# Moving per-head and per-batch vector work inside the attention stage of an attention and two-MoE kernel

## The chip, the cores and the metric

One Trainium2 chip, one of its cores. The metric is the device time of the kernel in microseconds; a run is one execution. The kernel before was run three times; one execution was profiled.

## The reference

Attention over q, k, v of shape [4 batches, 8 heads, 1152, 64] with queries pooled by two, and then two mixture-of-experts layers over the 2304 resulting rows of 512:

```python
q_pool = q.reshape(B, H, S // 2, 2, D).mean(axis=3)
scores = scale * np.matmul(q_pool, k.transpose(0, 1, 3, 2))
scores = scores - np.max(scores, axis=-1, keepdims=True)
attn = np.exp(scores)
attn = attn / (np.sum(attn, axis=-1, keepdims=True) + 1e-09)
x = rows(np.matmul(attn, v))                 # 2304 x 512, heads side by side
# layer 1: rows with x @ w_skip > 0 get x + gate * relu(x @ w1[e]) @ w2[e], e = argmax(x @ w_gate)
# layer 2: every row gets gate * sigmoid(x @ w_output_gate)[e] * relu(x @ w1[e]) @ w2[e]
```

Each layer has 8 experts of 1024 hidden units.

## The kernel before

The kernel has an attention stage over 32 heads (to about 575 us) and then two MoE stages that run tiles of 128 rows sorted by expert. The change is in the attention stage alone.

**Bodies.** Every engine runs one program order, `body(h)` for h from -2 to 32. In body h different heads are in different states: keys and queries of head h+2 are transposed and split into a high and a low part, the row maximum of head h+1 is found, the exact scores and exponentials of head h are made, and head h-1 is multiplied with the values, summed, transposed back and divided.

**PE (TensorE).** In body h, for each of nine key tiles t: `scores(h, t, half)` (L566, L567), and beside them the fifteen `prior(h+1, b)` blocks (L553), a coarse product of 384 columns whose maximum DVE takes. Priors use two banks in turn, so prior b waits until DVE has reduced block b-2. At t=0, 2 and 4 stand the twelve matmuls of `weighted(h-1, group)` (L583), at t=4 also `sums(h-1)`, at t=5 and 6 the transposes and small products back (L605, L611, L620), and at t=7 `trans_ql(h+1)` (L539, its transposes recorded at L501), which waits for `neg_max`. `ranks_of_batch(b)` (L632 to L641) counts, for a finished batch, how many rows go to each expert; it shares a bank with `weighted`, so `weighted` waits for routing step 8 (L579).

**ACT (ScalarE).** `exps(h, t)` (L848) after each score tile, the split of keys and queries, and, at t=7, after exp 7, the two copies `ql_out` (L859) that the next head's scores wait for.

**POOL (GpSimd).** `accumulate(h)` (L440, L443) adds the nine exponential tiles of head h in eight additions of 128x576, each after its exp, so that the additions of head h run partly during body h+1. After it, in the bodies named in SCATTER_IN, two indirect DMAs (`scatter_rows`, L457) send finished rows of a batch to memory.

**DVE (VectorE).** `pool_q(h+2)` (L1009), fifteen `block_max(h+1, b)` (L1035), between them `k_low` (L1015 to L1021: parts 0 and 1 after block 1, part 2 after block 5) and `q_low` (L1028, after block 7), then `negate_max(h+1)` (L1040) and `divide(h-1)`: den (L1048), reciprocal (L1050), tmpL (L1054), xrow (L1059) and, last, the addition of tmpL to the routing logits L (L1063). Each increments `norm`; five increments a head.

**Routing steps.** When a batch's eight heads are done (body RANKS_IN[b] = 9, 17, 25 for batches 0 to 2), eighteen small DVE steps (`route_step`, L1065) choose experts, gates and target rows. Each waits for the step ahead of it (`rt_chain`). RT_GAPS says where they stand: (late, place): [steps] is, in body RANKS_IN[b]+late, after block `place` (5 or 9; NBLK is the end of the body). Batch 3 has all its steps behind the last body. The names by line are: step 0 L1076 to L1078, 1 L1080 and L1082, 2 L1084, 3 L1088, 4 L1090, 5 L1093, 6 L1095, 7 L1097 and L1098, 8 L1102, 9 L1105 and L1106, 10 L1108 and L1109, 11 L1113, 12 L1115, 13 L1118, 14 L1121, 15 L1123, 16 L1125 and L1126, 17 L1128.

Of the kernel before, what the change touches and what calls it, by code (L numbers as in the profile page):

```python
# [5 lines left out]
def attention_moe_moe(nc, q, k, v, w_skip, w_gate1, w1a, w2a, w_gate2, w_ogate, w1b, w2b, out):  # L6
# [13 lines left out]
    PN = 128  # L20


    B, H, S, D = q.shape
    NH = B * H
# [3 lines left out]
    QT = -(-SQ // PN)  # L28
    Q_LAST = SQ - (QT - 1) * PN
    KB_ = 384  # L30
    NB = S // KB_
    NBLK = QT * NB
# [4 lines left out]
    TB = 2 * OJ  # L37
# [27 lines left out]
    with ctx:  # L65
# [156 lines left out]
        MXB, SB, OB, TR = 0, 2, 6, 7  # L222
# [38 lines left out]
        def tiles_of(ap, odd):  # L261
# [4 lines left out]
        RANKS_IN = [(b + 1) * H + 1 for b in range(B - 1)]  # L266
        RT_STEPS = 18
        RT_CHAIN = RT_STEPS - 1
        RT_GAPS = {(0, 5): [0], (0, 9): [1], (1, 5): [2, 3], (1, 9): [4], (2, 5): [5], (2, 9): [6, 7], (2, NBLK): [8],
                   (3, 5): [9], (3, 9): [10], (4, 5): [11, 12], (4, 9): [13, 14], (5, 5): [15], (5, 9): [16, 17]}  # L270
        SCATTER_IN = {at + 5 + n: (b, range(2 * n, 2 * n + 2)) for b, at in enumerate(RANKS_IN) for n in range(TB // 2)}

        def has(g):
            return 0 <= g < NH
# [224 lines left out]
        def _(pe):  # L499
            def transpose(o, i, n=PN):  # L500
                return nc.tensor.transpose(o, i, ident[0:n, 0:n])  # L501
# [31 lines left out]
            def trans_ql(g, j):  # L533
                u = g % 2
                if j == 0:
                    pe.wait_ge(neg_max, g + 1)
                for t in range(3 * j, min(QT, 3 * j + 3)):
                    o = (t % 3) * PN
                    last = transpose(PS[0:D + 1, MXB + j, o:o + PN], QLN[u][:, t, 0:D + 1])  # L539
                last.then_inc(qlt_done, 1)  # L540

            def prior(g, b):
# [28 lines left out]
            def weighted(g, group):  # L571

                u = g % 2
                if group == 0:
                    pe.wait_ge(v_in[u], 16 * nth(g))
                    wait(pe, norm, HEAD_NORM * (g - 1) + 3)
                    for b, at in enumerate(RANKS_IN):
                        if g == at + 2:
                            pe.wait_ge(rt_chain, b * RT_CHAIN + 9)  # L579
                pe.wait_ge(exp_done, KT * g + 3 * group + 3)  # L580
                for t in range(3 * group, 3 * group + 3):
                    for half in range(2):
                        last = nc.tensor.matmul(PS[64 * half:64 * half + D, OB, 0:HQ], Vt[u][:, t, :],  # L583
                                                P[u][:, t, half * HQ:(half + 1) * HQ],
                                                start=(t == 0), stop=(t == KT - 1))
                if group == 2:
                    last.then_inc(pv_done, 1)
# [58 lines left out]
            def body(h):  # L646

                now, after, before = has(h), has(h + 1), has(h - 1)
                blocks = iter(range(NBLK))
                for t in range(KT):  # L650
                    if t == 3 and has(h + 2):
                        trans_qh(h + 2, 0)
                    if now:
                        scores(h, t, 0)
                    if after and t < 7:
                        prior(h + 1, next(blocks))
                    if after and t < 7 and h <= 0:
                        keep_busy(1)
                    if now:
                        scores(h, t, 1)  # L660
                    if after and t < 7:
                        prior(h + 1, next(blocks))
                    if after and t < 7 and h <= 0:
                        keep_busy(2 if h < 0 else 1)
                    if t == 0:
                        if has(h + 2):
                            trans_k(h + 2, 0)
                            if h == FIRST:
                                keep_busy(14)
                        if before:  # L670
                            weighted(h - 1, 0)
                    if t == 1 and has(h + 2):
                        trans_k(h + 2, 1)
                        if h == FIRST:
                            keep_busy(5)
                    if t == 2 and before:
                        weighted(h - 1, 1)
                    if t == 3 and has(h + 2):
                        if h == FIRST:
                            keep_busy(5)  # L680
                        trans_qh(h + 2, 1)
                        if h == FIRST:
                            keep_busy(4)
                    if t == 4:
                        if before:
                            weighted(h - 1, 2)
                            sums(h - 1)
                        if after:
                            prior(h + 1, next(blocks))
                    if t == 5 and before:  # L690
                        back_values(h - 1)
                    if t == 6 and h - 2 in RANKS_IN:
                        ranks_of_batch(RANKS_IN.index(h - 2))
                    if t == 6 and before:
                        back_sums(h - 1)
                        back_logits(h - 1)
                    if t == 7 and after:
                        trans_ql(h + 1, 0)
                        trans_ql(h + 1, 1)
# [109 lines left out]
        def _(act):  # L809
# [101 lines left out]

            for h in range(FIRST, LAST):
                body(h)
                if h - 2 in RANKS_IN:
                    route_exps(RANKS_IN.index(h - 2))
            route_exps(B - 1)

            def route_acts(i):
# [56 lines left out]
        def _(dve):  # L975
# [67 lines left out]
            def divide(g):  # L1043

                T = PS[0:OP, TR, 0:OJ * PN].rearrange("p (j a d) -> p j a d", j=OJ, a=2)
                dve.wait_ge(out_done, g + 1)
                both = PS[0:OP, TR, OJ * PN:OJ * (PN + 2)]
                vec.tensor_scalar(den[:, :], both, 1e-9, None, ALU.add).then_inc(norm, 1)  # L1048
                dve.wait_ge(norm, HEAD_NORM * g + 1)
                vec.reciprocal(rden[:, :], den[:, :]).then_inc(norm, 1)  # L1050
                dve.wait_ge(norm, HEAD_NORM * g + 2)
                b, c = g // H, (g % H) * D
                by = rden[:, :].rearrange("p (j a) -> p j a", a=2).unsqueeze(3)
                vec.tensor_tensor(tmpL[:, :, :, :], PS[0:OP, OB, LOG:LOG + OJ * 2 * NL]  # L1054
                                  .rearrange("p (j a n) -> p j a n", j=OJ, a=2),
                                  by.broadcast_to([OP, OJ, 2, NL]), ALU.mult).then_inc(norm, 1)
                if b >= 2 and g % H == 0:
                    dve.wait_ge(rt_scat[b % 2], 16 * TB * (b // 2))
                vec.tensor_tensor(xrow[b % 2][:, :, c:c + D].rearrange("p (a j) d -> p j a d", a=2), T,  # L1059
                                  by.broadcast_to([OP, OJ, 2, D]), ALU.mult).then_inc(norm, 1)  # L1060
                dve.wait_ge(norm, HEAD_NORM * g + 3)
                Lb = L[:, b * TB:(b + 1) * TB, :].rearrange("p (a j) n -> p j a n", a=2)
                vec.tensor_tensor(Lb, Lb, tmpL[:, :, :, :], ALU.add).then_inc(norm, 1)  # L1063
# [78 lines left out]
                        ins.then_inc(w_lo[m], 1)  # L1142

            def body(h):
                routing = [(late, b) for b, at in enumerate(RANKS_IN) for late in range(6) if h == at + late]

                def route_in(place):
                    for late, batch in routing:
                        for n in RT_GAPS.get((late, place), ()):
                            route_step(batch, n)  # L1150
                if has(h + 2):
                    pool_q(h + 2)
                for b in range(NBLK):
                    if has(h + 1):
                        block_max(h + 1, b)
                    if has(h + 2):
                        if b == 1:
                            k_low(h + 2, 0)
                            k_low(h + 2, 1)
                        if b == 5:  # L1160
                            k_low(h + 2, 2)
                        if b == 7:
                            q_low(h + 2)
                    route_in(b)
                if has(h + 1):
                    negate_max(h + 1)
                if has(h - 1):
                    divide(h - 1)
                route_in(NBLK)
# [4 lines left out]
                body(h)  # L1174


            for done, n in enumerate([*range(8), *range(11, 17), 8, 9, 10, 17]):
                route_step(B - 1, n, done)

# [153 lines left out]
```

## Time and profile before

| | |
|---|---|
| runs | 1157.24, 1161.58, 1158.62 us; median 1158.62 |
| profiled execution | 1157.24 us, its span 1155.5 us |
| PE, DVE, ACT, POOL busy | 96%, 64%, 46%, 39% of the span |
| granted TensorE clock, mean | 0.983 |
| chain that ended last | PE 84%, DVE 5%, ACT 4% |

The span runs from the first to the last instruction; the time of a run lies a little above it. Times inside the profile are microseconds from the span's start. A row of a timeline gives start, length (from the first start to the last end for several, "x2"), engine, line, operation, and in brackets how long the engine stood idle before it and what released it. Successive DVE operations overlap in their records by about 0.08 us.

### The profile page before, as it was taken

What the parts mean: (1) busy time and instruction counts of PE and PEld (TensorE: products, weight loads), DVE (VectorE), ACT (ScalarE), POOL (GpSimd) and SP (SyncE); (2) the same over time, 40 slices, a digit from 0 to 9 for tenths busy, and PEclk for the clock granted to TensorE, in tenths of its full rate; (3) what the DMA queues carried; (4) which work ended last, traced back from release to release, by engine and by line L of the source; (5) the groups of instructions that cost most, each with busy time, mean ns of one, the idle gap of its engine ahead of it and who ended that gap; (6) DMA issues with size and microseconds to landing.
All of it is one profiled execution on the core that took longest, in us unless ns stands there. A gap on an engine that the chain in (4) does not pass through costs nothing.

```text
span 1155.5 us, 22128 instructions
## 1 busy us (share of the span) xinstructions
PE 1105.6 (96%) x7821; PEld 931.7 (81%) x7821; DVE 740.0 (64%) x1706; ACT 534.6 (46%) x945; POOL 454.1 (39%) x339
## 2 busy tenths in 40 slices
PE   7999999999999999999879999999799999999996
PEld 5777777777777777777578899988689999999995
DVE  7766667787678766776336777676545556555641
ACT  3555655555555555554323444443143534453320
POOL 0768876767876678666710000000000010000100
PEclk9999999999999999999989999999889999999999
DMA  5262225223332234211458214275492472141100
GB/s 128 65 225 73 62 73 145 63 73 86 76 87 72 63 86 100 68 47 38 158 176 319 111 37 174 79 268 185 174 341 91 157 277 97 38 172 36 46 10 14
DMA packets 74398, 132.61 MB, mean 115 GB/s; under 512 B 11040, under 2 KB 29472, under 8 KB 74320
## 3 DMA queue, kind: packets, MB, share of 16 engines
q10 hardware_dynamic: 26240, 69.22, 16.6%
q1 hardware_dynamic: 43424, 50.58, 16.4%
q0 software_dynamic: 4656, 11.79, 2.9%
q8 instruction: 46, 0.75, 0.3%
q14 instruction: 32, 0.26, 0.1%
HBM read 106.12 MB, written 19.24 MB: 108 GB/s over the span
## 4 chain that ended last, share of the span: by engine, by line
PE 84%; DVE 5%; ACT 4%; issue 2%; DMA 2%; ACTq 1%; POOL 1%; SPq 0%; DVEq 0%; POOLq 0%
PE PS L732 20%; PE PS L583 13%; PE PS L553 9%; PE PS L566 7%; PE PS L501 7%; PE PS L749 6%; PE PS L567 6%; PE PS L745 6%; PE PS L746 6%; ACT arena_p L848 2%; ACT QLT L859 2%; DVE W2L L1139 2%; PE PS L620 1%; PE PS L596 1%; PE PS L764 1%
## 5 line engine op out<-in xcount | busy, mean ns | idle before, releaser
L443 POOL TENSOR_TENSOR arena_a<-arena_a,arena_p 128x576 f32<-128x576 f32 x224 | 334.0, 1491 | 94.0 <-ACT arena_p L848 75.1
L1035 DVE TENSOR_REDUCE mx<-PS 128x1 f32<-128x384 f32 (+1 forms) x480 | 246.7, 551 | 120.6 <-PE PS L553 117.2
L732 PE MATMUL PS<-moe,W 128*128 128x128 f32 x2432 | 281.4, 277 | 2.2 <-ACT moe L934 2.2
L732 PEld LDWEIGHTS PS<-moe,W 128*128 128x128 f32 x2432 | 278.5, 193 | 4.6 <-ACT moe L934 2.8
L848 ACT ACTIVATE arena_p<-PS 128x576 f32<-128x576 f32 x288 | 187.6, 653 | 151.1 <-PE PS L567 150.3
L566 PE MATMUL PS<-QHT,KA 128*128 128x288 f32 x576 | 191.2, 335 | 7.6 <-ACT QLT L859 7.6
L553 PE MATMUL PS<-KA,QHT 128*128 128x384 f32 (+1 forms) x480 | 173.3, 362 | 2.1 <-DVE mx L1035 2.0
L567 PE MATMUL PS<-QLT,KB 65*128 65x288 f32 x576 | 168.8, 297 | 0.0
L820 ACT CAST W2H<-W2R 128x1024 fp32r<-128x1024 f32 x148 | 144.3, 1048 | 51.4 <-PE PS L749 40.7
L1139 DVE TENSOR_TENSOR W2L<-W2R,W2H 128x1024 fp32r<-128x1024 f32 x144 | 166.5, 1218 | 1.5 <-ACT W2H L820 1.5
L583 PE MATMUL PS<-arena_p,arena_a 128*64 128x288 f32 x1152 | 160.5, 414 | 0.0
L491 POOL DMA_INDIRECT out<-moe,oidx x23 | 22.8, 990 | 293.7 <-DVE moe L1299 293.7
L566 PEld LDWEIGHTS PS<-QHT,KA 128*128 128x128 f32 x576 | 109.3, 190 | 32.2 <-ACT QLT L859 14.9
L954 ACT ACTIVATE hTh<-PS 128x512 fp32r<-128x512 f32 x76 | 45.3, 597 | 191.1 <-PE PS L732 191.1
L745 PE MATMUL PS<-W2H,hTh 128*128 128x512 f32 x304 | 123.6, 406 | 1.4 <-ACT hTh L954 1.4
L746 PE MATMUL PS<-W2L,hTh 128*128 128x512 f32 x304 | 119.0, 392 | 0.0
L583 PEld LDWEIGHTS PS<-arena_p,arena_a 128*64 128x64 f32 x1152 | 74.4, 136 | 55.2 <-issue 16.8
L567 PEld LDWEIGHTS PS<-QLT,KB 65*128 65x128 f32 x576 | 109.3, 190 | 0.0
L474 POOL DMA_INDIRECT xs<-moe,tpu x16 | 18.0, 1124 | 225.7 <-DVE tpu L1258 225.7
L553 PEld LDWEIGHTS PS<-KA,QHT 128*128 128x128 f32 (+1 forms) x480 | 86.2, 180 | 25.3 <-issue 13.1
L749 PE MATMUL PS<-W2H,hTl 128*128 128x512 f32 x304 | 82.8, 394 | 2.4 <-DVE hTl L1218 2.4
L501 PE MATMUL PS<-ident,arena_a 128*128 128x128 f32 (+2 forms) x480 | 81.2, 278 | 3.7 <-DVE KA L1021 2.1
(174 smaller groups left out, 1174.1 us busy)
## 6 DMA issues: line engine op xcount, KB each, us to landing
W<-in_moe_w ACTq DMA_DIRECT2D x16, 2048.0 KB, 14.5
W2R<-in_moe_w ACTq DMA_DIRECT2D x16, 2048.0 KB
moe<-xs SPq DMA_DIRECT2D x40, 258.0 KB, 2.7
arena_a<-in_k SPq DMA_DIRECT2D x32, 288.0 KB, 2.9
arena_a<-in_v SPq DMA_DIRECT2D x32, 288.0 KB, 2.8
KB<-KA SPq DMA_DIRECT2D x32, 288.0 KB
arena_a<-in_q SPq DMA_DIRECT2D x32, 256.0 KB, 3.2
xs<-padrow SPq DMA_DIRECT2D x8, 258.0 KB, 3.2
```

Of the source, the lines that this page charges most:

```text
L443: nc.gpsimd.tensor_tensor(Acc[u], Acc[u], P[u][:, t, :], ALU.add).then_inc(acc_step, 1)
L501: return nc.tensor.transpose(o, i, ident[0:n, 0:n])
L553: nc.tensor.matmul(PS[0:n, MXB + b % 2, 0:KB_], QHT[g % 3][:, t * PN:t * PN + n], KA[g % 3][:, c * KB_:(c + 1) * KB_], start=True, stop=Tr ...
L566: nc.tensor.matmul(o, KA[g % 3][:, t * PN:(t + 1) * PN], QHT[g % 3][:, cols], start=True, stop=False)
L567: last = nc.tensor.matmul(o, KB[u][:, t * PN:(t + 1) * PN], QLT[u][:, cols], start=False, stop=True)
L583: last = nc.tensor.matmul(PS[64 * half:64 * half + D, OB, 0:HQ], Vt[u][:, t, :], P[u][:, t, half * HQ:(half + 1) * HQ], start=(t == 0), st ...
L732: last = nc.tensor.matmul(PS[:, HB + f // 4, (f % 4) * PN:(f % 4 + 1) * PN], W1[s][:, d, f * PN:(f + 1) * PN], xT[:, d, :], start=(d == 0) ...
L745: nc.tensor.matmul(PS[:, YB, 0:DM], hTh[:, f, :], W2H[s][:, f, :], start=(f == 0), stop=False)
L746: nc.tensor.matmul(PS[:, YB, 0:DM], hTh[:, f, :], W2L[s][:, f, :], start=False, stop=False)
L848: nc.scalar.activation(P[u][:, t, :].rearrange("p (a c) -> p a c", a=2), PS[:, b:b + 2, 0:HQ], ACT.Exp, scale=SCALE).then_inc(exp_done, 1)
L1035: vec.reduce_max(mx3[0:n, t, c:c + 1], PS[0:n, MXB + b % 2, 0:KB_], AX.X).then_inc(pr_max, 1)
L1139: ins = vec.tensor_tensor(W2L[s][:, f, :], W2R[s][:, f, :], W2H[s][:, f, :].bitcast(f32), ALU.subtract)
```

## The change

There are four edits, all in the attention stage.

1. `trans_ql` transposes the last query tile with its 64 real rows instead of 128.
2. The addition of a head's logits to L leaves `divide`, and becomes `add_logits(g)`; it runs one body later, after block 5 of the maxima (after `k_low` part 2 and ahead of the routing steps there). The last head's runs behind the last body, ahead of batch 3's steps.
3. The routing steps of batches 0 to 2 stand in four bodies instead of six; PE's ranks, its wait in `weighted` and ACT's `route_exps` come one body earlier.
4. The scatter pairs of a batch come two bodies earlier.

```diff
-        RT_GAPS = {(0, 5): [0], (0, 9): [1], (1, 5): [2, 3], (1, 9): [4], (2, 5): [5], (2, 9): [6, 7], (2, NBLK): [8],
-                   (3, 5): [9], (3, 9): [10], (4, 5): [11, 12], (4, 9): [13, 14], (5, 5): [15], (5, 9): [16, 17]}
-        SCATTER_IN = {at + 5 + n: (b, range(2 * n, 2 * n + 2)) for b, at in enumerate(RANKS_IN) for n in range(TB // 2)}
+        RT_GAPS = {(0, 5): [0], (0, 9): [1, 2, 3], (1, 5): [4, 5], (1, 9): [6, 7], (1, NBLK): [8], (2, 5): [9],
+                   (2, 9): [10], (3, 5): [11, 12], (3, 9): [13, 14, 15, 16, 17]}
+        SCATTER_IN = {at + 3 + n: (b, range(2 * n, 2 * n + 2)) for b, at in enumerate(RANKS_IN) for n in range(TB // 2)}
...
                 for t in range(3 * j, min(QT, 3 * j + 3)):
+                    n = PN if t < QT - 1 else Q_LAST
                     o = (t % 3) * PN
-                    last = transpose(PS[0:D + 1, MXB + j, o:o + PN], QLN[u][:, t, 0:D + 1])
+                    last = transpose(PS[0:D + 1, MXB + j, o:o + n], QLN[u][0:n, t, 0:D + 1], n)
...
                     for b, at in enumerate(RANKS_IN):
-                        if g == at + 2:
+                        if g == at + 1:
                             pe.wait_ge(rt_chain, b * RT_CHAIN + 9)
...
-                    if t == 6 and h - 2 in RANKS_IN:
-                        ranks_of_batch(RANKS_IN.index(h - 2))
+                    if t == 6 and h - 1 in RANKS_IN:
+                        ranks_of_batch(RANKS_IN.index(h - 1))
...
-                if h - 2 in RANKS_IN:
-                    route_exps(RANKS_IN.index(h - 2))
+                if h - 1 in RANKS_IN:
+                    route_exps(RANKS_IN.index(h - 1))
...
                                   by.broadcast_to([OP, OJ, 2, D]), ALU.mult).then_inc(norm, 1)
+
+            def add_logits(g):
+
+                b = g // H
                 dve.wait_ge(norm, HEAD_NORM * g + 3)
                 Lb = L[:, b * TB:(b + 1) * TB, :].rearrange("p (a j) n -> p j a n", a=2)
                 vec.tensor_tensor(Lb, Lb, tmpL[:, :, :, :], ALU.add).then_inc(norm, 1)
...
-                routing = [(late, b) for b, at in enumerate(RANKS_IN) for late in range(6) if h == at + late]
+                routing = [(late, b) for b, at in enumerate(RANKS_IN) for late in range(4) if h == at + late]
...
+                    if b == 5 and has(h - 2):
+                        add_logits(h - 2)
                     route_in(b)
...
+            add_logits(NH - 1)
             for done, n in enumerate([*range(8), *range(11, 17), 8, 9, 10, 17]):
                 route_step(B - 1, n, done)
```

## Rows read from the trace of the kernel before

**Rows 1.** The page, part 4: the chain that ended last, by engine.

```profile
PE 84%; DVE 5%; ACT 4%; issue 2%; DMA 2%; ACTq 1%; POOL 1%; SPq 0%; DVEq 0%; POOLq 0%
```

**Rows 2.** The timeline of all engines around the end of one head.

```profile
311.86 0.71 PE L501 MATMUL PS<-ident,arena_a 128*65 128x128 f32 x5
312.06 0.65 ACT L848 ACTIVATE arena_p<-PS 128x576 f32<-128x576 f32 x1 [1.11 <-PE PS L567]
...
312.57 0.30 DVE L1063 TENSOR_TENSOR L<-L,tmpL 96x150 f32<-96x150 f32 x1
312.61 0.68 ACT L859 CAST QLT<-PS 65x384 fp32r<-65x384 f32 x2
...
313.34 0.40 PE L566 MATMUL PS<-QHT,KA 128*128 128x288 f32 x1 [0.23 <-ACT QLT L859]
...
314.10 1.02 DVE L1035 TENSOR_REDUCE mx<-PS 128x1 f32<-128x384 f32 x2 [0.82 <-PE PS L553]
```

**Rows 3.** DVE's timeline over that head, with steps 0 and 1.

```profile
311.08 0.17 DVE L1040 TENSOR_REDUCE arena_a<-mx 128x5 fp32r<-128x15 f32 x1
...
319.37 0.28 DVE L1021 TENSOR_TENSOR KA<-PS,KA 64x128 fp32r<-64x128 f32 x1
319.69 0.20 DVE L1076 TENSOR_SCALAR do<-L 96x6 f32<-96x6 f32 x1
...
321.32 1.02 DVE L1035 TENSOR_REDUCE mx<-PS 128x1 f32<-128x384 f32 x2 [1.20 <-PE PS L553]
322.25 0.48 DVE L1028 TENSOR_TENSOR arena_a<-arena_a 128x320 fp32r<-128x320 f32 x1
...
323.59 0.53 DVE L1080 TENSOR_TENSOR gex<-L,gmx 96x96 f32<-96x96 f32 x1
...
325.34 1.59 DVE L1035 TENSOR_REDUCE mx<-PS 128x1 f32<-128x384 f32 x3 [1.05 <-PE PS L553]
...
328.20 0.17 DVE L1040 TENSOR_REDUCE arena_a<-mx 128x5 fp32r<-128x15 f32 x1
```

**Rows 4.** POOL's timeline, from four heads.

```profile
227.17 3.03 POOL L443 TENSOR_TENSOR arena_a<-arena_a,arena_p 128x576 f32<-128x576 f32 x2 [0.53 <-ACT arena_p L848]
...
234.16 1.44 POOL L443 TENSOR_TENSOR arena_a<-arena_a,arena_p 128x576 f32<-128x576 f32 x1
...
251.28 1.42 POOL L443 TENSOR_TENSOR arena_a<-arena_a,arena_p 128x576 f32<-128x576 f32 x1
...
318.43 1.42 POOL L440 TENSOR_TENSOR arena_a<-arena_p 128x576 f32<-128x576 f32 x1
...
322.31 1.69 POOL L443 TENSOR_TENSOR arena_a<-arena_a,arena_p 128x576 f32<-128x576 f32 x1 [0.90 <-ACT arena_p L848]
...
324.14 1.42 POOL L443 TENSOR_TENSOR arena_a<-arena_a,arena_p 128x576 f32<-128x576 f32 x1
```

**Rows 5.** DVE's timeline: routing steps in other heads and in the tail.

```profile
225.10 0.17 DVE L1040 TENSOR_REDUCE arena_a<-mx 128x5 fp32r<-128x15 f32 x1
...
227.33 1.60 DVE L1009 TENSOR_TENSOR arena_a<-arena_a 128x320 f32<-128x320 f32 x1
...
234.25 1.38 DVE L1106 TENSOR_TENSOR Racc<-Racc,Rsum 96x16 f32<-96x16 f32 x1
...
242.58 0.17 DVE L1040 TENSOR_REDUCE arena_a<-mx 128x5 fp32r<-128x15 f32 x1
...
251.48 1.24 DVE L1115 TENSOR_SCALAR gden<-gden 96x12 f32<-96x12 f32 x1
...
336.81 0.25 DVE L1084 TENSOR_TENSOR gc<-gc,rev 96x96 f32<-96x96 f32 x1
...
577.51 0.17 DVE L1115 TENSOR_SCALAR gden<-gden 96x12 f32<-96x12 f32 x1
```

**Rows 6.** PE's weight loads ahead of prior blocks 8 and 12.

```profile
321.93 0.19 PEld L553 LDWEIGHTS PS<-KA,QHT 128*128 128x128 f32 x1
...
325.95 0.13 PEld L553 LDWEIGHTS PS<-KA,QHT 128*64 128x64 f32 x1 [0.18 <-DVE mx L1035]
```

## The prediction

> **What bounds the kernel now.** The page comes first [rows 1]: on one core, the chain of work that ended last runs on PE for 84% of the span. The edits touch only the attention stage, up to about 575 us, so the next view is DVE's timeline. From one negate_max (L1040) to the next are 17.12 us [rows 3]. That period repeats through the stage, except for three heads of 17.48 us, which follow the ranks on PE (225.10 to 242.58, one of three) [rows 5]. So a routing step costs the kernel nothing today; only the rank matmuls cost 0.36 us a batch, and they stay.
>
> Next, what sets 17.12 us. At the end of a head [rows 2] PE issues scores(7) and then, from 311.86, the five transposes of trans_ql. ACT starts exp(7) at 312.06, released by scores(7), and starts the two QLT copies at 312.61, behind exp(7). The next head's first score waits for them until 313.34. This path runs through ACT, and the transposes are beside it. Inside a head PE issues without a break, with one stop: prior block 12 waits 0.18 us for the block maximum of block 10, the one that starts at 325.34 [rows 6]. Block 8 goes out at 321.93, when the maximum of block 6 (321.32, about 0.55 us long) has just ended at 321.87. At those two blocks DVE has no slack: what it is late there, PE is late, and nothing after it in the body gives time back. DVE's own room is ahead of them: 1.20 us idle before block maximum 6 with step 0 in it, 1.05 us before block maximum 10 with step 1 in it [rows 3]. These are the places (5) and (9) of the routing table.
>
> Last, POOL. Its adds of 1.42 us stand at fixed places in a head, as ACT's exps release them [rows 4]. Rows show what they do to DVE. Step 12 (L1115), 96x12, takes 1.24 us at 251.48, until POOL's add of 251.28 ends at 252.70; the same step took 0.17 us in the tail (577.51), where POOL is idle. L1009, 128x320 with two inputs, takes 1.60 us at 227.33, behind the add of 227.17; L1028, of the same size, takes 0.48. L1080 takes 0.53 us and ends when the add of 322.31 has ended; L1084, of the same size, takes 0.25 with no add beside it. The maxima, whose input lies in PSUM, never stretch [rows 3 to 5]. So a DVE operation with two SBUF inputs, or a copy or tensor_scalar in SBUF, stands still till the running add ends. Which side wins a tie is seen too: L1028 at 322.25 wins against the add of 322.31, which is stretched to 1.69 us; L1106 at 234.25 loses against the add of 234.16 and takes 1.38 us [rows 3 to 5].
>
> **The shorter transposes.** One of a head's five transposes has 64 columns instead of 128. The five take 0.47 us until the next LDWEIGHTS, 0.09 each; so the saving is 0 to 0.05 us a head [rows 2]. It lies ahead of scores(8), after which PE waits for QLT anyway: 0. Only in the first two heads does PE wait for L1040, so below 0.1 us in all.
>
> **The L addition moved from divide to place 5.** It leaves some 0.22 us of the head's end free (0.30 us less the overlap of 0.08). What follows on DVE is L1009 and then 0.82 us of idle time until PE's first prior [rows 2]: gain 0. In the tail it stands in the same place of the chain. At place 5 it starts when DVE is free of k_low(2), 319.37+0.28, so 8.61 us after L1040 with a gap of 0.04 us, like L1076 now. POOL's second add starts at 8.70 (251.28 - 242.58): L gets in ahead of it, ends at 8.9, and the room holds it in the 20-odd heads without routing. Cost 0; if it loses, it ends 0.18 us after the add's 10.12, which is 0.06 late.
>
> **The routing table.** Body at+n is body h = RANKS_IN[b] + n. I lay the steps on one head, times from L1040, with the slots that rows give [rows 3, 4]. Place 5 opens at 8.61, and block maximum 6 is due at 10.24. Place 9 opens at 12.51 and block maximum 10 is due at 14.26. POOL runs 8.8-10.2 (pushed a little by L), 11.23-12.9, 13.06-14.48, then nothing until 15.7. Gaps behind a wait are 0.04 us and an operation starts 0.08 us before the end of the one ahead if nothing separates them.
>
> Body at+0. Place 5: L, then step 0, whose first instruction waits for L and so comes at 8.95, into the second add. Released at 10.2, step 0 ends at 10.45, block maximum 6 starts at 10.39: 0.15 late. Then L1028 starts at 11.32, after POOL's third add (11.23): by the L1106 tie it loses, waits until about 12.65 and, with 0.34 after the release (L1009: 228.93 against 227.17 + 1.42), ends at 13.0. Block maxima 8 and 9 follow, 0.46 us each, still in time for priors 10 and 11, which have 1.7 us of room; place 9 opens at 13.85 instead of 12.51. POOL's fourth add, now 12.8-14.27, holds step 1. Steps 1, 2 and 3 then run freely, each about 0.25 (L1084) and 0.04: block maximum 10 starts at 15.03 instead of 14.26, **0.77 us late**. If L1028 wins instead, step 2 (L1084, two SBUF inputs) comes at 13.23, just after the fourth add, and is held to 14.48: then 0.55 at place 9 beside 0.1 at place 5, almost the same.
>
> Body at+1. L, then step 4 is held to 10.2 and step 5 waits for it: block maximum 6 is 0.29 late; L1028 loses; place 9 opens at 13.85 and takes step 6 (held to 14.27) and step 7 (two reduces): maximum 10 at 14.76, **0.50 late** over both places. Before, steps 6 and 7 fitted. Step 8 at the end is L1102 with L1009 behind it, as before.
>
> Body at+2. Step 9 behind L: L1105 held, maximum 6 0.09 late; step 10 alone at place 9: **0.10**.
>
> Body at+3. Steps 11 and 12: L1113 is a reduce, L1115 is held as now, no delay. Place 9 takes 13 to 17. Step 13 ends at 12.94, step 14 at 13.20, step 15 (L1123) comes at 13.24 and is held by the fourth add to 14.50; steps 16 and 17, at 0.17 an instruction by the tail's L1115, take 0.4 more: maximum 10 at 14.89, **0.63 late**, and 0.90 if L1028 loses here too (its margin is 0.06 us). I take 0.65.
>
> Sum: 0.77 + 0.50 + 0.10 + 0.65 = 2.02 us a batch, three batches, 6.06 us, less under 0.1 us of prologue: 6.0 us. Ends: 0 if these steps are never held (steps 2 and 3 would add 0.57 us to a room that has 1.05), and, if L1028 loses its tie in all four bodies and pushes the fourth add to end at 14.4, with the four bodies' steps behind that, 0.91 + 0.59 + 0.28 + 1.02 = 2.8 us a batch, 8.4 in all.
>
> One term hangs on whether step 0's L1076, a strided tensor_scalar, is held at all. The row leaves it open: 0.20 us at 319.69, POOL's add of that head ending at 319.85 [rows 3, 4]. I take it as held, like L1115, the nearest row; if it is not, body at+0 costs 0.55 and the sum is 5.3.
>
> The Trainium skill, "SBUF — State Buffer", section "SBUF: two separate sides", says that VectorE and GpSimd share a pair of SBUF ports under an exclusive lock, which an operation in a two-port mode or with two SBUF inputs takes for its whole length. By that rule L1076 is held too and the sum is the 6.0; by the other reading of the row it is 5.3. The trace agrees with the rule in L1115 and L1106.
>
> **Ranks, exps, scatters.** They keep their distance to the steps. PE's ranks still come after step 5 with 6 us to spare, route_exps still between steps 7 and 11. Scatter pairs move two bodies up. The pair in body 30, which stands in front of the last head's eight adds, is still there, only from another n: the last chain through POOL is not shortened. The pairs of bodies 31 and 32 vanish from beside the final divide, whose operations run at their usual lengths there today (L1063 0.30): under 0.1 us.
>
> **Rivals.**
> Hidden: DVE is not held, or PE makes it up. For: 1.05 and 1.20 us of idle time at the places, and no step now moves the 17.12. Against: the held rows and PE's 0.18 us wait at block 12. Time: 1157.2, chance 0.25.
> Slower: L1028 loses its tie in body at+3 too, and every step with a two-input operation meets an add. One mechanism, POOL's add ahead of DVE at q_low; it decides from 0.06 us of delay at block maximum 6. 8.4 us: 1165.6, chance 0.25. Against: L1115 alone ended in time for 252.82.
> Faster: the L addition and the transpose are on the path after all. 32 x (0.22 + 0.05) = 8.6 us: 1148.6. Against: both lie beside waits that end later; chance 0.03.
>
> **How the numbers follow.** The profiled execution took 1157.24 us (span 1155.5), the lowest of the three; their median is 1.4 above it. 1157.24 + 6.0 = 1163.2, chance 0.47, its own range 1161 to 1165. With the hidden and the held case the range is 1157 to 1166.5. A measurement tells about 0.5%, 5.8 us, from no change: from the median that is 1152.8 to 1164.4. Slower: the held case and a quarter of my own, 0.37. Faster 0.03. Same 0.60.
>
> **What would show it.** L1040 to L1040: 17.12 in bodies without routing; longer by about 0.8, 0.5, 0.1 and 0.65 in the four bodies of a batch (plus the ranks' 0.36 after at+1). L1084, L1123, L1090 and L1105 stretched beside a POOL add; L1028 at 1.5 us or more in at+0 and at+1; PE's idle time before block 12 rising from 0.18 to over 0.6; L1063 at 0.30. The prediction is wrong if PE's wait before block 12 stays at 0.18, or if L1063 itself is stretched in every head.

## The result and the profile after

The changed kernel takes 1163.89 us (median of 7 runs, 1162.94 to 1165.81) against 1158.59 us for the kernel before (7 runs, 1156.15 to 1161.58). The ratio is 1.0051, with a 95% interval of 1.0036 to 1.0065: slower, by 5.3 us between the medians and by 5.9 us by the ratio. The forecast was 1163.2 us with a range of 1157 to 1166.5. The profiled execution took 1163.63 us, its span 1161.9.

Where the time went is read from the starts of the 32 `negate_max` operations (L1040, now L1041), as for [rows 3]. From head 2 to head 31 they lie 496.87 us apart before (53.91 to 550.78) and 502.36 us apart after (53.93 to 556.29): 5.49 us in the attention stage. The rest of the span's 6.4 us lies behind it. The load of the first MoE stage's second tile of rows (L397, issued by SyncE) is issued at 599.11 before and 604.71 after, 5.60 us, and the remaining 0.8 us is within what single runs of either kernel differ by. All but 0.04 of the 5.49 us lies in the twelve bodies that hold routing steps; in the other heads from 3 to 30 the period is 17.11 to 17.14 us in both kernels.

First the page's part 4, the chain that ended last, to be set beside [rows 1]:

```profile
PE 82%; DVE 11%; issue 2%; DMA 2%; POOL 1%; SPq 0%; DVEq 0%; ACTq 0%; ACT 0%; POOLq 0%
```

ACT has left the chain (4% before) and DVE has 11% instead of 5%. Part of that is the real delay and part is a quirk of the head's end, told below.

DVE's timeline in the body at+0 of batch 0, to be set beside [rows 3] (lines have moved: negate_max is L1041, the maxima L1036, q_low L1029, L is added at L1068, step 0 is L1081 to L1083, step 1 L1085 and L1087, step 2 L1089, step 3 L1093):

```profile
173.82 0.17 DVE L1041 TENSOR_REDUCE arena_a<-mx 128x5 fp32r<-128x15 f32 x1
...
182.42 0.31 DVE L1068 TENSOR_TENSOR L<-L,tmpL 96x150 f32<-96x150 f32 x1
182.77 1.27 DVE L1081 TENSOR_SCALAR do<-L 96x6 f32<-96x6 f32 x1
...
184.19 1.00 DVE L1036 TENSOR_REDUCE mx<-PS 128x1 f32<-128x384 f32 x2
185.12 0.47 DVE L1029 TENSOR_TENSOR arena_a<-arena_a 128x320 fp32r<-128x320 f32 x1
...
187.18 1.35 DVE L1089 TENSOR_TENSOR gc<-gc,rev 96x96 f32<-96x96 f32 x1
188.57 0.25 DVE L1093 TENSOR_REDUCE gcm<-gc 96x12 f32<-96x96 f32 x1
188.74 1.57 DVE L1036 TENSOR_REDUCE mx<-PS 128x1 f32<-128x384 f32 x3
...
191.59 0.17 DVE L1041 TENSOR_REDUCE arena_a<-mx 128x5 fp32r<-128x15 f32 x1
```

POOL's adds beside it, as in [rows 4]:

```profile
182.52 1.49 POOL L443 TENSOR_TENSOR arena_a<-arena_a,arena_p 128x576 f32<-128x576 f32 x1
...
185.05 3.38 POOL L443 TENSOR_TENSOR arena_a<-arena_a,arena_p 128x576 f32<-128x576 f32 x2 [1.04 <-ACT arena_p L849]
```

The reader is to see three things. L1081, a 96x6 tensor_scalar, lasts 1.27 us and ends at 184.04, when the add of 182.52 has ended at 184.01. Step 2's L1089, a 96x96 product of 0.25 us, lasts 1.35. And where the row of block maximum 10 had 1.05 us of idle time in front of it before, here it has none: it starts 14.92 us after negate_max instead of 14.26. PE's weight loads ahead of prior block 12, in the bodies at+0, at+1 and at+3, tell what this costs, beside 0.18 in [rows 6]; the second row is prior block 8 in the body at+1:

```profile
189.34 0.13 PEld L554 LDWEIGHTS PS<-KA,QHT 128*64 128x64 f32 x1 [0.72 <-DVE mx L1036]
...
202.70 0.19 PEld L554 LDWEIGHTS PS<-KA,QHT 128*128 128x128 f32 x1 [0.23 <-DVE mx L1036]
...
206.91 0.13 PEld L554 LDWEIGHTS PS<-KA,QHT 128*64 128x64 f32 x1 [0.36 <-DVE mx L1036]
...
242.21 0.13 PEld L554 LDWEIGHTS PS<-KA,QHT 128*64 128x64 f32 x1 [0.81 <-DVE mx L1036]
```

In the body at+1 the delay comes in two parts: prior 8 goes out 11.11 us after negate_max instead of 10.84, 0.27 us late, and the wait at block 12 adds 0.18. The chain of holds is the longest there. DVE's timeline: step 4 (L1095) behind L, q_low (L1029) behind POOL's third add, and the two maxima behind q_low:

```profile
200.42 1.47 DVE L1095 TENSOR_TENSOR gc<-gc,gcm 96x96 f32<-96x96 f32 x1
...
203.03 1.55 DVE L1029 TENSOR_TENSOR arena_a<-arena_a 128x320 fp32r<-128x320 f32 x1
204.50 1.01 DVE L1036 TENSOR_REDUCE mx<-PS 128x1 f32<-128x384 f32 x2
```

The periods from one negate_max to the next, for the four bodies of batch 0 (batches 1 and 2 give the same to 0.03 us):

| body | before | after | after - before | forecast |
|---|---|---|---|---|
| at+0 | 17.12 | 17.77 | +0.65 | +0.77 |
| at+1 | 17.12 | 17.57 | +0.45 | +0.50 |
| at+2 | 17.11 | 17.54 | +0.07 and the ranks' 0.36, which came one body later before | +0.10 |
| at+3 | 17.48 | 17.76 | +0.64 without that 0.36 | +0.65 |

These sum to 1.81 us a batch, 5.4 in three.

### The profile page after: what moved, and what is told of

Its sections match the earlier page's. It is cut to its first block, busy times and chain, and to the rows that moved or that the text cites. A ratio compares the mean times of both kernels' runs of the same rounds, so it can differ in the third digit from the quotient of the medians.

```text
span 1161.9 us, 22128 instructions
## 1 busy us (share of the span) xinstructions
PE 1116.4 (96%) x7821; PEld 934.7 (80%) x7821; DVE 752.0 (65%) x1706; ACT 537.6 (46%) x945; POOL 451.3 (39%) x339
## 4 chain that ended last, share of the span: by engine, by line
PE 82%; DVE 11%; issue 2%; DMA 2%; POOL 1%; SPq 0%; DVEq 0%; ACTq 0%; ACT 0%; POOLq 0%
PE PS L733 20%; PE PS L584 10%; PE PS L501 8%; PE PS L567 8%; PE PS L554 7%; PE PS L750 6%; PE PS L746 6%; PE PS L568 6%; PE PS L747 6%; DVE mx L1036 3%; PE PS L621 1%; DVE W2L L1144 1%; PE PS L765 1%; PE PS L612 1%; PE PS L597 1%
## 5 line engine op out<-in xcount | busy, mean ns | idle before, releaser
L1036 DVE TENSOR_REDUCE mx<-PS 128x1 f32<-128x384 f32 (+1 forms) x480 | 246.3, 550 | 111.6 <-PE PS L554 108.5
L567 PE MATMUL PS<-QHT,KA 128*128 128x288 f32 x576 | 191.8, 337 | 0.5 <-ACT QLT L860 0.5
L567 PEld LDWEIGHTS PS<-QHT,KA 128*128 128x128 f32 x576 | 109.2, 190 | 25.3 <-issue 14.5
L501 PE MATMUL PS<-ident,arena_a 128*128 128x128 f32 (+3 forms) x480 | 84.3, 278 | 4.0 <-DVE KA L1022 2.1
```

Of the source, the lines that this page charges most:

```text
L567: nc.tensor.matmul(o, KA[g % 3][:, t * PN:(t + 1) * PN], QHT[g % 3][:, cols], start=True, stop=False)
L1036: vec.reduce_max(mx3[0:n, t, c:c + 1], PS[0:n, MXB + b % 2, 0:KB_], AX.X).then_inc(pr_max, 1)
```

## The experiments

Each run's stage time below is from the negate_max of head 2 to that of head 31: 496.87 us in the kernel before. In the two kernels below whose heads should take as long as before it comes out at 496.85 and 496.86, so it tells apart what medians of runs, which spread over 1 to 6 us, can't. It is one profile of each kernel, and the seventeen heads that hold no routing steps sum to up to 0.11 us less in two of the runs, though nothing in them should differ: a stage time is good to about 0.1 us. Medians are given with the kernel before on the same chip; ratios have their 95% intervals.

**Only the routing table.** `RT_GAPS`, the ranks, `route_exps` and the scatters as in the change, on the kernel before.

```diff
-  RT_GAPS = {(0, 5): [0], (0, 9): [1], (1, 5): [2, 3], ...
+  RT_GAPS = {(0, 5): [0], (0, 9): [1, 2, 3], (1, 5): [4, 5], ..., (3, 9): [13, 14, 15, 16, 17]}
-  SCATTER_IN = {at + 5 + n: ...
+  SCATTER_IN = {at + 3 + n: ...
```

> The kernel before with the routing table, the ranks, route_exps and the scatters of the change; the L addition and the transposes stay as before. Held-behind-POOL theory: place 5 is as in the kernel before, so block maximum 6 is late in no body; at place 9 step 2 (body at+0) and step 15 (body at+3) come just behind POOL's fourth add and are held about 1.3 us each. The bodies cost +0.55, 0, 0 and +0.63 us, 3.5 us in all over the attention stage. Rival, that packing costs by the number of instructions: body at+3, with seven instructions at place 9 against two before, would cost clearly more than at+0 with four, and none would show a stretched L1084 or L1123.

Measured: 1161.58 against 1158.21 us, ratio 1.0035 (1.0018 to 1.0052); stage 500.11, +3.24 us. The bodies cost +0.54, 0, 0 and +0.60. DVE's timeline has the held step 2 and step 15, and the steps around them at their usual length:

```profile
186.68 1.36 DVE L1084 TENSOR_TENSOR gc<-gc,rev 96x96 f32<-96x96 f32 x1
188.07 0.25 DVE L1088 TENSOR_REDUCE gcm<-gc 96x12 f32<-96x96 f32 x1
...
238.91 1.26 DVE L1123 TENSOR_TENSOR gw<-gw,do 96x12 f32<-96x12 f32 x1
240.21 0.17 DVE L1125 COPY arena_x<-idx_f 96x6 f32<-96x6 f32 x1
```

The six instructions at place 9 of at+3 cost 0.06 us more than the four of at+0: the number of instructions is not what costs, one held operation in each body is.

**Only the L addition.**

```diff
+            def add_logits(g):
...
+                    if b == 5 and has(h - 2):
+                        add_logits(h - 2)
                     route_in(b)
```

> The kernel before with only the L addition moved to place 5, routing over six bodies as before. Held theory: nothing in bodies without routing (17.12 us each). In body at+0 step 0 waits for L and is held, block maximum 6 about 0.13 late; at+1 step 2 is held behind L and step 3 follows, about 0.2 late; at+2 to at+5 at most 0.06 each. Some 0.4 us a batch, 1.2 us in all. Rival, that the addition is a gain at the head's end: every period falls below 17.12. Rival, that it loses the tie with POOL's second add everywhere: every period grows by up to 0.06 us and L1063 is about 1.5 us long.

Measured: 1160.42 against 1158.21 us, ratio 1.0013 (0.9999 to 1.0027), alone not told from no change; stage 498.14, +1.27 us. Bodies at+0 and at+1 have periods of 17.24 and 17.38 (+0.12 and +0.26), the others up to 0.06 more. Heads without routing stay at 17.12: the addition wins its tie in all heads but the last (0.30 to 0.31 us long, 0.55 there) and gains nothing by having left divide.

Alone the two edits cost 3.24 and 1.27 us, 4.5 together; the change costs 5.49. Of the 0.98 us left over, about 0.2 lies in the heads without routing steps, which are 0.1 us shorter in either run than before; the twelve routing bodies by themselves give 3.35, 1.37 and 5.45 us, so the interaction is 0.73 us. Of it 0.18 us a batch is in at+1: there the addition pushes q_low behind POOL's third add, so place 9 opens 1.35 us late, which steps 6 and 7 no longer fit, while one step 4 did.

**Only the shorter transpose.**

```diff
+                    n = PN if t < QT - 1 else Q_LAST
-                    last = transpose(PS[0:D + 1, MXB + j, o:o + PN], QLN[u][:, t, 0:D + 1])
+                    last = transpose(PS[0:D + 1, MXB + j, o:o + n], QLN[u][0:n, t, 0:D + 1], n)
```

> The kernel before with only the transpose of 64 rows. In the changed kernel the weight load of the 64-row transpose starts 0.17 us late and scores(8) goes out 0.26 us later than before, relative to the head. Theory: the short transpose costs PE about 0.26 us a head, all of it hidden in PE's wait for QLT, which falls from 0.39 us to 0.12 us: periods stay 17.12, time unchanged within 0.3 us. Rival, that it saves: scores(8) goes out earlier than 1.25 us after L1040.

Measured: 1157.78 against 1158.21 us, ratio 0.9997 (0.9981 to 1.0013); stage 496.85. PE's weight loads at the end of a head whose negate_max starts at 122.69:

```profile
123.33 0.49 PEld L501 LDWEIGHTS PS<-ident,arena_a 128*65 128x65 f32 x4
123.99 0.13 PEld L501 LDWEIGHTS PS<-ident,arena_a 64*65 64x65 f32 x1 [0.17 <-issue]
124.19 0.19 PEld L567 LDWEIGHTS PS<-QHT,KA 128*128 128x128 f32 x1
...
124.94 0.19 PEld L567 LDWEIGHTS PS<-QHT,KA 128*128 128x128 f32 x1 [0.19 <-ACT QLT L860]
```

scores(8) goes out 1.50 us after negate_max instead of 1.24 (in the same head before, 123.61 with negate_max at 122.37): the shorter form costs 0.26 us, and it is hidden because PE waits for QLT right behind. PEld's wait for QLT falls from 0.47 to 0.19 us. This is also why ACT left the chain of the page (1% in this run, 4% in the run with only the routing table): PE now comes to the head's end so close to the QLT copies that the chain is followed through PE.

**The changed kernel with POOL's adds cut to 16 columns.** The output lacks most of the softmax sums.

```diff
-  nc.gpsimd.tensor_tensor(Acc[u], Acc[u], P[u][:, t, :], ALU.add).then_inc(acc_step, 1)
+  nc.gpsimd.tensor_tensor(Acc[u][:, 0:16], Acc[u][:, 0:16], P[u][:, t, 0:16],
+                          ALU.add).then_inc(acc_step, 1)
```

> The changed kernel with POOL's seven later additions of each head cut to 16 of 576 columns, so the softmax sums are not computed in full; the waits and the order stay. Held theory: step 2, step 4, step 9, step 15 and step 0 take 0.17 to 0.25 us each, block maxima 6 and 10 are on time in all four bodies, and the attention stage loses 5.4 us: periods of 17.12 everywhere but for the ranks' 0.36 us once a batch. Rival, that DVE's own instruction count or the waits between steps cost the time: periods of 17.6 to 17.8 remain in the routing bodies. The MoE stages may route otherwise and are not compared.

Measured, in one execution of 1159.19 us: stage 496.86 us, 5.50 less than the changed kernel and the time of the kernel before. Every period is 17.12, but for 17.48 once a batch. DVE's timeline, place 9 of at+0 and of at+3 again:

```profile
187.21 0.26 DVE L1090 TENSOR_TENSOR gc<-gc,rev 96x96 f32<-96x96 f32 x1
187.50 0.25 DVE L1094 TENSOR_REDUCE gcm<-gc 96x12 f32<-96x96 f32 x1
188.52 1.59 DVE L1037 TENSOR_REDUCE mx<-PS 128x1 f32<-128x384 f32 x3 [0.77 <-PE PS L555]
...
238.92 0.17 DVE L1129 TENSOR_TENSOR gw<-gw,do 96x12 f32<-96x12 f32 x1
```

With DVE's program unchanged, the whole loss is gone: it was POOL's adds that DVE stood behind. The ranks, `route_exps` and the scatters stand at the change's places here too, so their move costs nothing.

**The changed kernel with another table.** Steps 2, 3 and 15 to 17 go to the end of the body; still four bodies.

```diff
-  (0, 9): [1, 2, 3], (1, 5): [4, 5], ... (3, 9): [13, 14, 15, 16, 17]}
+  (0, 9): [1], (0, NBLK): [2, 3], (1, 5): [4, 5], ... (3, 9): [13, 14], (3, NBLK): [15, 16, 17]}
```

> The changed kernel with steps 2 and 3 of body at+0 and steps 15 to 17 of body at+3 taken from place 9 to the end of the body, behind divide, where DVE waits about 1 us for the next prior; still four bodies. Held theory: block maximum 10 is on time in at+0 and at+3, and those bodies cost only what place 5 leaves, about 0.1 and 0 us; at+1 stays at +0.45 and at+2 at +0.06. 0.6 us a batch, 1.9 us over the stage against 5.4 for the changed kernel. Rival, that the end of the body has no room: block maxima 0 to 3 come late and the two bodies stay at over 0.4 us each.

Measured: 1159.42 against 1158.81 us, ratio 1.0008 (0.9995 to 1.0022); stage 498.79, +1.92 us. The bodies cost +0.13, +0.44, +0.07 and 0. The end of the body is not free of holds (pool_q, L1010, lasts 1.56 us behind step 3), but there no prior waits for it.

**What sets the head's end.** If PE's wait for QLT hides the transposes' cost, taking the wait away must both gain time and bring the cost out. `back_sums` and `back_logits` were moved behind `scores(h, 7)`.

```diff
-                    if t == 6 and before:
+                    if t == 7 and before:
                         back_sums(h - 1)
                         back_logits(h - 1)
                     if t == 7 and after:
```

> The kernel before with back_sums and back_logits of head h-1 moved from ahead of scores(h, 7) to behind it, so that ACT's exp(7) starts about 1 us earlier and the QLT copies are ready when PE has done scores(8). Theory that the head's end is set by scores(7), exp(7) and the two QLT copies: PE's 0.39 us wait falls to about 0, the period from 17.12 to 16.7 to 16.8 us, 10 to 12 us over the stage, unless DVE's now later divide is held by a POOL add and eats 0.3 us of it. Rival, that PE's work sets the period: it stays 17.12.

Measured: 1159.72 against 1157.57 us, ratio 1.0023 (1.0005 to 1.0040); stage 497.88, +1.01. The expectation failed: the period is 17.05, not 16.7 to 16.8, and the body with the ranks has 18.47. Two new waits took the old one's place. From the timelines of PE's weight loads and of DVE, in the head whose negate_max starts at 121.63:

```profile
123.62 0.19 PEld L566 LDWEIGHTS PS<-QHT,KA 128*128 128x128 f32 x1 [0.26 <-ACT QLT L859]
...
128.31 0.19 PEld L553 LDWEIGHTS PS<-KA,QHT 128*128 128x128 f32 x1 [0.25 <-DVE mx L1035]
```

```profile
123.65 1.24 DVE L1063 TENSOR_TENSOR L<-L,tmpL 96x150 f32<-96x150 f32 x1
```

The QLT copies now wait for the transposes, which stand behind both back operations, and DVE's divide comes 0.5 us later, so that its two-input L addition falls behind a POOL add, and with it pool_q and the next four maxima.

**The same with the shorter transpose, and with a plain matmul of 64 columns.** The first adds the 64-row edit above; the second keeps 128-row weights:

```diff
+                        last = nc.tensor.matmul(PS[0:D + 1, MXB + j, o:o + n], QLN[u][:, t, 0:D + 1], ident[:, 0:n],
+                                                start=True, stop=True)
```

> The run with back_sums and back_logits late, and the 64-row transpose of the change besides. With PE's wait for QLT gone, a cost of the short transpose no longer hides. Theory, from the 0.26 us by which scores(8) is late in the changed kernel: the period is 0.15 to 0.26 us longer than in the run with the full transpose, 5 to 8 us over the stage. Rival, that the short form is cheaper: equal or up to 0.05 us shorter.

> The run with back_sums and back_logits late, with the last query tile transposed by a plain matmul of all 128 rows against 64 columns of the identity, so that 64 columns are written but the weights keep 128 rows. If the delay of the short transpose comes with its 64-row weights, scores(8) is not late here and the period is that of the run with the full transpose, within 0.05 us. If it comes with 64 columns, the period is as long as in the run with the short transpose.

Measured: 1156.08 and 1158.62 against 1157.57 us, ratios 0.9987 (0.9977 to 0.9997) and 1.0012 (0.9998 to 1.0026). Both have the period of 17.05 us, so the first theory's number did not come. PE's wait for QLT had not gone in the run with the full transpose: it was 0.26 us there, it is 0.20 with 64 columns and nothing with 64-row weights, so the short form just used it up and was hidden again. The place of scores(8) does tell them apart: 1.16 us after negate_max with the full transpose, 1.23 with 64 columns and 128-row weights, 1.44 with 64-row weights. So the delay comes with the 64-row form and not with the 64 columns. The run with 64 columns uses a plain matmul besides; a plain matmul with 64-row weights was not run. The short form's stage is even 3.8 us shorter than the full form's (494.11 against 497.88), 3.6 of it in the three bodies with the ranks (17.27 against 18.47): there exp(8) and POOL's last add come later, behind pool_q, which then takes 0.47 us instead of 1.70. That is again a tie with a POOL add, decided by chance of placement.

**The L addition with the back operations late.**

> The run with back_sums and back_logits late, and the L addition of the change at place 5, routing over six bodies. If DVE is late at the head's end there, because divide comes later and the two-input L addition and pool_q stand behind a POOL add, taking L away gives up to 0.3 us a head back, less 1.3 us over the stage for the routing steps held behind it. If DVE is in time there, the stage is 1.3 us longer than without the move.

Measured: 1153.35 against 1157.57 us, ratio 0.9966 (0.9951 to 0.9982); stage 492.80. The period is 16.93, 0.12 less than without the move, and the ranks' body falls from 18.47 to 17.31. Here, where DVE is late at the head's end, the same edit that cost 1.27 us gains 5.1. Of these, 3.5 us are the three bodies with the ranks, which the tie with the POOL add had made long.

**Both waits taken away.** On the kernel before: the L addition at place 5, the transposes between the two back operations, and `pool_q` of the next body right behind `negate_max`. The second run has the 64-row transpose besides.

```diff
+                    if t == 7 and before:
+                        back_sums(h - 1)
                     if t == 7 and after:
                         trans_ql(h + 1, 0)
                         trans_ql(h + 1, 1)
+                    if t == 7 and before:
+                        back_logits(h - 1)
...
                     negate_max(h + 1)
+                if has(h + 3):
+                    pool_q(h + 3)
                 if has(h - 1):
                     divide(h - 1)
```

> The kernel before with the L addition at place 5, back_sums behind scores(h, 7), then trans_ql, then back_logits, and pool_q of the next body right behind negate_max, where DVE waits 0.7 us. From the run with both back operations late: its QLT copies start only when the transposes behind back_logits are done (PE waits 0.26 us), and pool_q stands 1.1 us behind a POOL add, which makes block maxima 0 to 3 late. Both waits should go: the period falls from 16.93 to 16.6 to 16.75 us, 11 to 14 us less than before over the stage, faster than both kernels. If pool_q loses its tie at the new place, divide and the next maxima are late and the period stays at 16.9.

> The same with the 64-row transpose. With PE no longer waiting for QLT, its 0.26 us a head (0.17 ahead of its weight load, 0.09 behind) must show: period longer by 0.2 to 0.28 us, 6 to 8 us over the stage. If it stays hidden, PE still waits for QLT or for DVE.

Measured: 1149.72 us and 1154.95 us against 1158.81; ratios 0.9910 (0.9890 to 0.9929) and 0.9965 (0.9950 to 0.9979). The first is faster than both kernels. Its stage is 487.46 us, 9.4 less than before, with a period of 16.71 to 16.72; with the short transpose 494.35 and 16.97. The period is as expected, but the stage gains less than the 11 to 14 us: of the 11.7 us that 0.40 us a head make, 2.3 go in the routing bodies, which the L addition at place 5 makes longer (16.99 in at+1, 17.32 in at+0 of batches 1 and 2). From the timelines of the two, first DVE and PE's weight loads with the full transpose (negate_max at 120.73), where PE goes from scores(8) at 121.98 to the next head at 122.50 with no idle time:

```profile
120.84 0.49 DVE L1010 TENSOR_TENSOR arena_a<-arena_a 128x320 f32<-128x320 f32 x1
```

```profile
120.96 0.52 PEld L501 LDWEIGHTS PS<-ident,arena_a 128*65 128x65 f32 x5
121.45 0.61 PEld L620 LDWEIGHTS PS<-wrh,OT 128*96 128x96 f32 x6
...
122.50 0.19 PEld L566 LDWEIGHTS PS<-QHT,KA 128*128 128x128 f32 x1
```

and with the short one (negate_max at 121.66), where the loads of back_logits (L621) start 1.00 us after negate_max instead of 0.72:

```profile
122.47 0.13 PEld L501 LDWEIGHTS PS<-ident,arena_a 64*65 64x65 f32 x1 [0.17 <-issue]
122.66 0.58 PEld L621 LDWEIGHTS PS<-wrh,OT 128*96 128x96 f32 x6
```

The 64-row transpose costs 0.25 us of every period, 6.9 us in the stage, once nothing hides it.

## Why the prediction was right

- **The base.** That routing steps cost nothing before and that 17.12 us is set by scores(7), exp(7), the QLT copies and PE's own work held. The gain of the final version shows that this path was worth 0.4 us a head.
- **Holds behind POOL.** That a two-input DVE operation, or a tensor_scalar in SBUF, stands until POOL's add ends was right, and the run with thin adds shows it: 5.50 us back, none left. The open case, L1076 (now L1081), was held, 1.27 us long; so the sum with it held had the mechanism right, though the measured 5.49 us lies nearer to the other sum, 5.3, because of the tie told next. That a tensor_scalar in a two-port mode is blocked while a GpSimd operation holds the ports is what the Trainium skill says ("SBUF — State Buffer", section "SBUF: two separate sides"); the trace agrees with that 1.27 us.
- **The sum.** 6.0 us forecast, 5.49 measured in the stage: 2.02 us a batch against 1.81. At+1, at+2 and at+3 are right to 0.05 us. In at+1 PE's wait before block 12 is 0.36 us and not over 0.6, since 0.27 us are lost at prior 8 already, as the 0.29 of the working had it. For at+0 the forecast is 0.12 too high, because of a tie: q_low started 0.07 us after POOL's record (185.12 against 185.05) and still won, where I had it lose, 0.09 behind, as L1106 had. The other course, named beside it (0.55 at place 9 and 0.1 at place 5), is what came, and q_low at 1.5 us or more in at+0, a sign that was named, did not. Why it won is open. In at+1 q_low started 0.22 us behind the add and lost, as forecast.
- **The landing.** The forecast of 1163.2 us is 0.7 below the measured median, closer than its parts: it was built on 1157.24, the lowest of three runs and 1.35 below the median of seven, and its 6.0 us are 0.7 above the 5.3 between the two medians. The two errors partly cancel, which is luck.
- **A reading.** L1084 (336.81) is not a row with no add beside it: an add starts 0.09 us later, at 336.90. The row shows an operation that started first and kept its 0.25 us, which leaves the argument as it was.
- **The transposes.** "0 to 0.05 us a head" saved was wrong in sign: the short form costs 0.26 us. The step that gave 0 for the change was right only because of the wait behind it, so the prediction named the right cover for the wrong thing. The prediction did not use what the Trainium skill has on this: "TensorEngine Tiling (Array Packing)", section "Key Properties", says that a change of tiling mode drains TensorE, and its section "Available Configurations" lists 64-row tiles as other modes than 128-row ones. The trace fits that with 0.17 us of idle time ahead of the 64-row load and 0.09 behind it; that the 64-row transpose runs in another mode, and that the engine drains there, was not itself seen.
- **The L addition.** No gain at the head's end, cost only where steps stand behind it: right, 1.27 us alone.
- **Hidden, slower, faster.** The hidden case is refuted by L1089 and L1128. The held case, q_low losing in at+3 too, didn't come: there it started on time. The faster case did not either.
- **The chances.** The ratio, 1.0051, lies on the bound of 0.5% between "same" (0.60) and "slower" (0.37). The mechanism was forecast with too little trust: 0.47, and 0.25 for no hold at all, though rows of holds stood in the trace.

## What to carry to other kernels

Idle time on an engine is not room for any work: where VectorE's gap lies beside a GpSimd operation, an operation with two SBUF inputs, or a cast or tensor_scalar in SBUF, that is put into it and starts second lasts until that operation ends, and what counts is where its start falls relative to the other's, in hundredths of a microsecond when the two are close. So lay the steps on the other engine's timeline, and put reduces and operations with an input in PSUM there instead, or move the steps to a place where their delay is not waited for. Look too at what hides a cost: the shorter transpose seemed free only because PE waited behind it, and an edit that costs 1.3 us in one order of work gains 5 in another.

## What the runs showed of the hardware

- A transpose of 64 rows by 65 columns between 128-row ones costs more than one of 128 rows: the next weight load comes 0.26 to 0.29 us later, in six kernels, and the period grows by 0.25 us where nothing hides it. 64 columns under 128-row weights cost 0.07 more than the full transpose, as a plain matmul of two weight loads. Weights of 65 rows between 128-row ones (L567 before) show no such gap.
- While a GpSimd add ran, VectorE was held in operations with two SBUF inputs (L1089, 1.35 us against 0.26 with thin adds) and in a tensor_scalar in SBUF (L1081, 1.27 against 0.17). It was not held in a reduce of SBUF (L1118, 0.24 us at 235.55, inside the add of 235.40) nor in an operation with one input in PSUM (L1022, 0.28 us wherever it stood).
- In a tie no single margin decides. q_low (L1029) still gets ahead when it starts 0.07 us after the start in GpSimd's record (185.12 against 185.05), and GpSimd's adds are stretched then (3.38 us for two instead of 2.97). With the L addition at place 5 and the back operations late it won even at 0.17 us (456.42 against 456.25). L1106 lost at 0.09 us, q_low at 0.22, step 0's tensor_scalar at 0.07 (314.35 against 314.28, in the fastest run), and once the L addition at 0.01 (62.24 against 62.23, in the last run). What makes the difference was not found.
- A held operation ends 0.03 us after the add when it is small (L1081: 184.04 against 184.01), 0.11 us after it for 96x96 (L1095: 201.89 against 201.78) and 0.35 us after it for 128x320 (L1029: 204.58 against 204.23).
